# Starting every SBUF buffer of 256 bytes or more at a multiple of 256 bytes, in an attention, Fourier and feed-forward kernel

## The reference

```python
# stage 1: attention within hash buckets, 8 heads of 64, per batch
mask = q_bucket[:, :, :, None] == k_bucket[:, :, None, :]      # buckets: signs of q @ proj, k @ proj (6 bits)
attn = softmax(where(mask, scale * q @ k.T, -1e9));  x = attn @ v
# stage 2: Fourier mixing and a feed-forward layer of 2048
mixed = real(fft(fft(x, axis=1), axis=2));  u = x + mixed
un = (u - mean) / sqrt(var + 1e-6)
x = u + maximum(un @ w_ch1, 0) @ w_ch2
# stage 3: gated value with a causal convolution of 5 taps
gate = sigmoid(sum_k conv_w[k] * shifted(x, k));  out = (gate * (x @ w_val)) @ w_out
```

## The kernel before

| buffers | start mod 256 before |
|---|---|
| `ident`, `X`, `w1_stage`, `w2_stage`, `w1_hi`, `w1_lo`, `w2_hi`, `w2_lo`, the folded parts `x_odd_*`, `x_even_*` | 128 |
| `seq_tab`, `un1_hi`, `un1_lo`, `x2T_0`, `feat_cos_hi` | 192 |
| `x2T_1`, `row_fold`, `x_even`, `un` | 64 |
| `x_odd`, `q_a*`, `q_b*`, `k_a*`, `k_b*`, `bits_sb`, `codes`, `q_raw*`, `k_raw*` | 96 |
| `feat_cos_lo`, `parts` (in this order) | 224, 32 |
| `feat_sin_*`, `v_in`, `prob*`, `probT*`, `outT`, `un0_hi`, `un0_lo`, `y_hi`, `y_lo`, `h_hi`, `h_lo`, `wvo_hi`, `wvo_lo`, `wvo_stage`, `y_out`, `gv_hi`, `gv_lo` | 0 |

## Time and profile before

### The profile page before, as it was taken

How to read it: one execution, slowest core, us unless ns; L and a number is a source line. 1 busy time by engine, 2 the same in 40 slices (tenths; PEclk the granted TensorE clock), 3 DMA queues, 4 the chain that set the end, 5 groups by cost and what they waited for, 6 DMA issues and landing times.

```text
span 629.7 us, 11008 instructions
## 1 busy us (share of the span) xinstructions
PE 619.7 (98%) x3742; PEld 503.0 (80%) x3742; DVE 345.8 (55%) x587; ACT 317.8 (50%) x610; POOL 250.8 (40%) x213
## 2 busy tenths in 40 slices
PE   7899999999999999999999999999999999999998
PEld 3677776767776776989888888888888888888786
DVE  3978888788888785795211111126333333349820
ACT  4877777777787783464322222235322333444242
POOL 4544433334338764356233332328434443404140
PEclk9999999999999999999999999999999999999999
DMA  6932323323332020001221222620222221000202
GB/s 143 238 107 62 89 69 83 88 75 98 94 96 63 12 64 1 1 1 34 68 68 43 58 67 67 200 68 32 69 67 67 67 67 50 0 1 1 84 18 100
DMA packets 34267, 42.15 MB, mean 67 GB/s; under 512 B 3520, under 2 KB 22208, under 8 KB 34240
## 3 DMA queue, kind: packets, MB, share of 16 engines
q1 hardware_dynamic: 32272, 37.38, 20.4%
q0 software_dynamic: 1728, 4.02, 2.6%
q10 hardware_dynamic: 240, 0.39, 0.4%
HBM read 38.63 MB, written 3.15 MB: 66 GB/s over the span
## 4 chain that ended last, share of the span: by engine, by line
PE 91%; DVE 4%; ACT 2%; issue 1%; POOL 1%; ACTq 0%; POOLq 0%; DVEq 0%
PE banks L1597 21%; PE banks L1583 21%; PE banks L1379 12%; PE banks L1396 11%; PE banks L1446 10%; PE banks L1676 5%; PE banks L1419 2%; PE banks L1529 2%; PE banks L1660 2%; PE banks L1332 2%; DVE x_then_u_then_gate L1246 1%; PE banks L1466 1%; PE banks L1338 1%; PE banks L1454 1%; PE banks L1503 1%
## 5 line engine op out<-in xcount | busy, mean ns | idle before, releaser
L1159 DVE SCALAR_TENSOR_TENSOR h_lo<-banks,h_hi 128x512 fp32r<-128x512 f32 x64 | 35.3, 557 | 169.4 <-ACT h_hi L834 169.4
L1028 DVE TENSOR_REDUCE row_min<-banks 128x1 f32<-128x768 f32 x96 | 91.8, 957 | 31.9 <-PE banks L1379 31.1
L721 ACT ACTIVATE prob<-banks,row_min 128x768 f32<-128x768 f32 x96 | 87.0, 906 | 29.1 <-DVE row_min L1028 29.0
L1583 PE MATMUL banks<-unT_hi,w_hi 128*128 128x512 f32 (+1 forms) x256 | 86.6, 338 | 0.4 <-issue 0.2
L1583 PE MATMUL banks<-unT_hi,w_lo 128*128 128x512 f32 (+1 forms) x256 | 86.4, 337 | 0.0
L1583 PE MATMUL banks<-unT_lo,w_hi 128*128 128x512 f32 (+1 forms) x256 | 86.3, 337 | 0.0
L1446 PE MATMUL banks<-ident,prob 128*128 128x128 f32 x576 | 79.3, 273 | 1.4 <-ACT probT L350 1.4
L563 POOL TENSOR_TENSOR w_lo<-w_stage,w_hi 128x512 fp32r<-128x512 f32 x32 | 45.3, 1416 | 86.6 <-ACT w_hi L752 86.6
L1446 PEld LDWEIGHTS banks<-ident,prob 128*128 128x128 f32 x576 | 68.1, 140 | 6.7 <-issue 1.9
L834 ACT ACTIVATE h_hi<-banks 128x512 fp32r<-128x512 f32 x64 | 31.2, 490 | 79.5 <-PE banks L1583 79.5
L1396 PE MATMUL banks<-probT,v_in 128*64 128x384 f32 x384 | 69.0, 495 | 0.0
(11 more groups left out here) (157 smaller groups left out, 1191.3 us busy)
## 6 DMA issues: line engine op xcount, KB each, us to landing
w_stage<-in_moe_w_ch SPq DMA_DIRECT2D x64, 256.0 KB, 2.8
q_raw<-in_q SPq DMA_DIRECT2D x32, 192.0 KB, 3.3
k_raw<-in_k SPq DMA_DIRECT2D x30, 192.0 KB, 3.6
v_in<-in_v SPq DMA_DIRECT2D x16, 192.0 KB, 2.8
out<-y_out SPq DMA_DIRECT2D x12, 256.0 KB, 2.0
seq_tables_sb<-in_dft POOLq DMA_DIRECT2D x6, 386.0 KB, 3.4
wvo_stage<-in_moe_w_val SPq DMA_DIRECT2D x1, 1024.0 KB, 5.7
wvo_stage<-in_moe_w_out SPq DMA_DIRECT2D x1, 1024.0 KB, 8.4
```

The source lines that it names most:

```text
L721: act.activation(prob[s % 2][:, :, :], s_tile(s), ACT.Exp, bias=row_min[:, s:s + 1], scale=-1.0, accum_out=row_sum[:, s:s + 1]).then_inc(e ...
L1028: dve.tensor_reduce(row_min[:, s:s + 1], s_tile(s), AX.XY, ALU.min).then_inc(min_ready, 1)
L1159: dve.scalar_tensor_tensor(out=h_lo[:, slot, at:at + size], in0=h_bank[c], scalar=0.0, in1=h_hi[:, slot, at:at + size].bitcast(F32), op0=A ...
L1583: op = pe.matmul(h_bank[c], w_[:, slot, kb, :], x_[:, kb, at:at + size], start=(kb == 0 and m == 0), stop=(kb == KB - 1 and m == 2))
```

## The change

The helper that makes the buffers now asks for a start at a multiple of 256 bytes for each buffer with 256 bytes or more in a partition, and at a multiple of 32 for the smaller ones (as before). No instruction, wait, shape or order is changed.

```diff
+import math
+
...
     C0 = 512
+    LINE = 256
     C1 = S - C0
...
         def sb(name, shape, dt=F32, where=ctx):
-            return where.enter_context(nc.sbuf_tensor(name, shape, dt))
+            row = 4 * math.prod(shape[1:])
+            return where.enter_context(nc.sbuf_tensor(name, shape, dt, align_bytes=LINE if row >= LINE else 32))
```

## The result

The changed kernel takes 632.69 us in the median of 22 runs (631.83 to 634.1), the kernel before 631.61 us in 22 runs beside them (630.78 to 632.68). The ratio is 1.0017 with a 95% interval of 1.0011 to 1.0023: slower by 0.7 to 1.5 us. That is outside the stated range of 628.9 to 631.8 us, and on the other side of the forecast. The profiled execution took 632.64 us, with a span of 631.0 us against 629.7.

A forecast was written before the change was run, and what follows sets the result against it. TensorE's matmul distances were taken to bound the kernel; `ffn1` and values gave -0.41 us, all other terms 0, so 631.41 became 631.00 us profiled, 630.9 us in the median, range 628.9 to 631.8 us.

The forecast's parts named there:

- That the time is the sum of the distances of the matmul starts, and only those can change: TensorE, 98% busy: time is the distances between 3742 matmul starts; unchanged instructions matter only by altering these or exposing hidden work.
- `ffn1` and the values: Feed-forward and value matmuls: `ffn1` gains 0.48 us in batch 0, nothing in batch 1; batch 1 values lose 0.07 us.
- Attention: Scores matmuls and transposes, with the Fourier stage: no gain taken; 0.4 us was the bound for the scores.
- `ffn2`: Second feed-forward matmuls: no gain taken, block pace staying 4.20 to 4.22 us; bounds were no gain or 1.50 us.
- The prediction's own sign of being wrong: Wrong if TensorE's waits grow, or if pace and remainder turn out to be tied in `ffn2`.
- the distance of the two starts decides: Rival, feed-forward operands: 128 apart is slowest, so `ffn2` gains as well; 628.8 to 629.9 us, chance 0.32.
- A start at 0 is the bad one: Rival, fp32r matmuls with a changed remainder: buffers at one remainder could meet in memory; 1.5 us slower, 632.8 us, chance 0.09.
- ScalarE, VectorE, GpSimd and DMAs: Casts, other engine work and transfers: remainders make no difference on the path, 0; the `w_stage` landing may get shorter.
- The sum: All terms together: -0.41 us against the profiled 631.41 us, giving 631.00 us; 630.9 us for the median of runs.

## Why the prediction was wrong, step by step

*That the time is the sum of the distances of the matmul starts, and only those can change:* right. The instruction list and every other engine's durations stayed, and the loss was found in the distances.

*`ffn1` and the values:* right in mechanism and sign, and smaller. `ffn1` of batch 0 went to 4.18 us, batch 1 stayed, three values of batch 1 took 0.02 us more, where 0.05 were forecast. But 4.18 us came only in the later blocks of batch 0. The first blocks after the one at the start have transposes of batch 1 between them, and stayed at 4.20 to 4.22 us, so the gain was some 0.3 us and not 0.48.

*Attention:* right, nothing moved. The row of 0.70 us for four matmuls of scores is only one of two kinds, though: in many places of the chain four take 0.90 us (225 ns each), so at 132.37 us before and at 132.98 us after. Their operands are 0 apart before and after, at 96 and then at 0.

*`ffn2`:* this is the step that failed. I took no gain and bounded the term by nothing below and 1.50 us above; I left out a loss, without a reason that excludes one. The bound, 4.163 us, came from the values, which have the order of `ffn1`; their distance of 192 is a bad one for an order in which 512 and 256 columns take turns (4.23 us). I had written that no row shows `ffn2`'s order at another remainder, and did not conclude that the effect can then have either sign. It measured +0.02 us on each of the ten later blocks of batch 0 (0.01 on the first six) and +0.04 on each of 16 of batch 1, some 0.9 us where the sum had 0. The prediction's own sign of being wrong, pace and remainder tied in `ffn2`, is what came.

*The rivals:* "the distance of the two starts decides" was right in its first half: both operands moved together change nothing (all at 96), one of them moved changes the pace. It is not the whole cause, as the two rhythms at one distance show. Its second half, that the distance of 128 is the slow one, was wrong for `ffn2`, which is slower still at 0. "A start at 0 is the bad one" had the sign, and the wrong mechanism: starts at 96 do the same. Its evidence, 4.21 to 4.18 us, was the distance between 128 and 64.

*ScalarE, VectorE, GpSimd and DMAs:* right. No duration changed by more than 1 ns on the casts and the landing of `w_stage` stayed at 2.8 us. The rule of the Trainium skill on descriptors (DMA: Bandwidth & Descriptors, How a descriptor splits into AXI transactions) would have let it get shorter; that rule is stated for reads, and the side that moved here is written. The trace shows nothing of it: the landing stayed, and the packets of 512 bytes took 27 ns each in the mean before and after.

*The sum:* by the chain the feed-forward layer and what follows are 0.04 + 0.59 = 0.63 us longer; forecast were 0.41 less. This part repeats: from the first `ffn1` to the last matmul it is 344.23 us before, 344.87 and 344.94 us in the two profiles of the changed kernel. The measured 0.7 to 1.5 us hold this and something more. That remainder is not settled. The second measurement of the same kernel gave a ratio of 1.001, and there pace alone explains it. In the kernel with all large buffers but the feed-forward parts as before, the ratio was 1.0019, 1.15 us in the medians, at 0.70 us of pace: so a remainder of some 0.45 us came there with the load buffers where they were before, within an interval of about 0.6 us either way. The halved clock does not make it up either. Executions with a mean granted clock of 0.997 or less took about 1 us more, but they were 11 of 33 of the changed kernel and 15 of 65 of the kernel before in the two later measurements, which is worth some 0.1 us. That the load buffers at 0 make a late start or the drop of the clock more frequent was neither shown nor excluded.

Why a distance acts at all was not seen directly. While a matmul streams its moving operand the weights of the next one are read, both from SBUF, and it would fit that the two reads get in each other's way; this is a guess that no run here tests. The Trainium skill (TensorE: Matmul & The Clock Gate, Step-by-step: what each phase is for) says the opposite: the two operands have read ports of their own, and loading weights takes nothing from the running matmul. By it one would expect one pace at all eight distances; measured were 4.16 to 4.24 us, so here the measurement decides that the distance matters, but it does not tell by what mechanism.

## What to carry to other kernels

Where TensorE is the bound and loads weights for each matmul, the place of its two operands relative to each other can count: here up to 2% of the time of `ffn2`. A round start address was worth nothing in itself. Changing the size of one unrelated buffer moves all that follow against those in front, so differences of some 0.2% after such an edit may be placement: compare the distances of matmul starts, block by block, before giving a reason. A cost bounded by a row of another order of shapes has to be bounded on both sides, and when a good distance is wanted it is tried with the real order, in the real loop.

## What the runs showed of the hardware that I had not expected

In the steady loops the distances of the matmul starts repeat from iteration to iteration within 1 or 2 ns, and come back as closely in another kernel with the same distance of the operands and the same order, whatever else lies where: all at 0 and all at 96 have the same 24 steps. For `ffn2` the pace goes from 4.16 to 4.24 us for 24 matmuls with the distance, 3.84 us being the columns alone. The same loop at the same distance can run in two rhythms, 4.17 and 4.21 us, in the two batches of one execution. And near the start the granted clock was 0.50 for 3.4 us in five of 14 profiles: in four it fell between 13.6 and 13.9 us, each time about 1 us after a wait of 1.8 us for GpSimd had ended, and in one (h at 32) at about 10 us, behind two shorter waits of 1.0 and 0.3 us. Five other profiles have a wait of 1.7 or 1.8 us too and kept the full clock.
